# Attention score products issued half a tile ahead, with GpSimd's and the loads' order rearranged

## The reference, cut to what matters

```python
# 1. attention, 8 heads of 64: keys in a band of 96 behind the query, and the first 8 keys
scores = q @ k.T / 8 - slope[head] * dist;  scores = where(keep, scores, -1e9)
a = exp(scores - max);  x = (a / sum(a)) @ v
# 2. gated product with a causal convolution of 5 taps
gate = sigmoid(sum_k conv_w[k] * x shifted by 4 - k);  x2 = (gate * (x @ w_val)) @ w_out
# 3. x2 @ w_in (1024 wide), relu, 3 taps, gate, @ moe2_w_out (1024 x 512)
h = relu(x2 @ w_in);  out = (h * sigmoid(conv3(h))) @ w2
```

## Time and profile before

| what | value |
|---|---|
| median of 3 runs | 260.68 us (260.28 to 261.41) |
| profiled execution, its own time | 260.86 us |
| its span, first to last instruction | 259.1 us |
| busy: PE, DVE, ACT, POOL | 96%, 71%, 57%, 18% of the span |
| TensorE clock granted | full in every slice |

### The profile page before, as it was taken

One profiled execution on the slowest core, in us unless ns is written; L12 is line 12 of the kernel. 1 busy time (PEld: TensorE's weight loads), 2 busy tenths in 40 slices (PEclk: granted clock), 3 DMA queues, 4 the chain that ended last, 5 costly groups with the idle time before them and its releaser, 6 DMA issues.

```text
span 259.1 us, 4771 instructions
## 1 busy us (share of the span) xinstructions
PE 248.1 (96%) x1702; PEld 199.7 (77%) x1702; DVE 183.4 (71%) x469; ACT 147.8 (57%) x346; POOL 46.8 (18%) x71
## 2 busy tenths in 40 slices
PE   8999989989789899999999999999999999999995
PEld 7644558888688778888888888888888888888883
DVE  0388369998989988989805969986139989990000
ACT  1061649999999854455517058855458559662100
POOL 1002255777478612000000000000000000000000
PEclk9999999999999999999999999999999999999999
DMA  6799957897976120000000000000000004004021
GB/s 204 266 341 270 287 199 202 248 239 229 271 220 202 57 74 4 0 4 0 0 0 3 0 0 0 1 3 0 0 0 3 0 0 162 3 0 162 0 115 47
DMA packets 24636, 24.69 MB, mean 95 GB/s; under 512 B 3732, under 2 KB 16532, under 8 KB 24484
## 3 DMA queue, kind: packets, MB, share of 16 engines
q1 hardware_dynamic: 23460, 23.37, 29.8%
q10 hardware_dynamic: 1152, 1.01, 1.2%
HBM read 21.03 MB, written 3.34 MB: 94 GB/s over the span
## 4 chain that ended last, share of the span: by engine, by line
PE 84%; ACT 9%; DVE 5%; issue 2%
PE ps L592 21%; PE ps L594 21%; PE ps L593 21%; PE ps L478 9%; ACT prob L732 6%; PE ps L559 3%; DVE prob L982 3%; PE ps L525 2%; PE ps L563 2%; ACT probT L739 2%; PE ps L493 2%; PE ps L489 1%; DVE probT L989 1%; DVE xT L1005 1%; ACT Wh L720 0%
## 5 line engine op out<-in xcount | busy, mean ns | idle before, releaser
L732 ACT ACTIVATE prob<-prob,low 128x232 f32<-128x232 f32 (+1 forms) x96 | 44.2, 465 | 4.9 <-DVE low L982 4.8
L1010 DVE SCALAR_TENSOR_TENSOR g<-xT,cw,g 128x512 f32<-128x512 f32 x48 | 34.7, 787 | 1.6 <-ACT g L767 1.6
L838 ACT ACTIVATE h<-ps 128x512 f32<-128x512 f32 x24 | 14.0, 596 | 31.2 <-PE ps L594 31.1
L982 DVE CUSTOM_DVE_ANT_0 prob<-ps,bias 128x232 f32<-128x232 f32 x80 | 28.0, 388 | 1.5 <-PE ps L525 1.5
L559 PE MATMUL ps<-probT,v_new 128*64 128x128 f32 x192 | 19.3, 280 | 6.5 <-ACT probT L739 6.5
L592 PE MATMUL ps<-gh,Wh 128*128 128x512 f32 x64 | 24.9, 389 | 0.0
L593 PE MATMUL ps<-gl,Wh 128*128 128x512 f32 x64 | 24.9, 389 | 0.0
L594 PE MATMUL ps<-gh,Wl 128*128 128x512 f32 x64 | 24.9, 389 | 0.0
L592 PE MATMUL ps<-hghA,w2h 128*128 128x512 f32 x64 | 24.9, 389 | 0.0
L593 PE MATMUL ps<-hglA,w2h 128*128 128x512 f32 x64 | 24.9, 389 | 0.0
L594 PE MATMUL ps<-hghA,w2l 128*128 128x512 f32 x64 | 24.9, 389 | 0.0
(11 more groups left out here) (110 smaller groups left out, 590.1 us busy)
## 6 DMA issues: line engine op xcount, KB each, us to landing
q_rows<-in_q SPq DMA_DIRECT2D x12, 256.0 KB, 4.3
kW<-in_k SPq DMA_DIRECT2D x12, 256.0 KB, 5.4
v_new<-in_v SPq DMA_DIRECT2D x12, 240.0 KB
invT<-inv_turned SPq DMA_DIRECT2D x20, 128.0 KB, 3.4
out<-xT SPq DMA_DIRECT2D x5, 512.0 KB, 2.8
w<-in_w SPq DMA_DIRECT2D x8, 256.0 KB, 9.3
v_old<-in_v SPq DMA_DIRECT2D x10, 192.0 KB
prob<-in_wval SPq DMA_DIRECT2D x1, 1024.0 KB, 4.9
```

Source lines behind the costliest of these rows:

```text
L732: act.activation(part, part, ACT.Exp, scale=-1.0, bias=low[:, t % 2, i:i + 1], accum_out=total[:, t % 2, i, 0:1]).then_inc(exp_done, 1)
L838: act.activation(h_cols(m, c), pieces(HB(m), c), ACT.Relu).then_inc(relu_done, 1)
L982: dve.tensor_tensor_reduce(prob[:, t % 2, i, cols], SC(f, e)[:, i % HH // 2, cols], table, -SCALE, 3.0e38, ALU.add, ALU.min, low[:, t % 2, ...
L1010: dve.scalar_tensor_tensor(out=pieces(g[:, m, :], c), in0=x_cols(m, c, tap - PAD1), scalar=cw1[:, m, tap:tap + 1], in1=pieces(g[:, m, :], ...
```

## The change

PE computes each half of a tile's scores half a tile ahead: in iteration t, after `turn(t)`, comes the first half of `qk(t+2)`, then `pv(t)`, then the second half of `qk(t+2)`. DVE's order follows: it scores the first half of tile 1 ahead of the loop, and begins iteration t with tile t's first copy, then `inverse(t)`, the other copy, `turn_inverse(t)`, the second half of tile t+1's scores, the first half of tile t+2's, and `take_x(t)` in the same iteration. The first two taps move from ACT to GpSimd (`first_taps`, as `tensor_scalar` from SBUF to SBUF, once, in iteration 5), and DVE's early steps from iterations 8, 9, 10 to 6, 7, 10. GpSimd runs `scale_x(t-1)` ahead of `key_window(t+3)`, and splits two rows of `w2` in iterations 0 and 1, one in each of 2 to 5. SP loads rows 0 to 3 of `w2` ahead of the loop, and rows 4 to 7 behind `spread_inverse(0)` to `spread_inverse(3)`.

```diff
-EARLY_STEPS = {t: 1 for t in range(TAPS_FROM + 3, TILES - 1)}
+EARLY_STEPS = {t: 1 for t in (TAPS_FROM + 1, TAPS_FROM + 2, TILES - 2)}
+W2_FIRST = 4
+W2_ROWS = {0: (0, 1), 1: (2, 3), 2: (4,), 3: (5,), 4: (6,), 5: (7,)}
...
-                for k in range(FT):
+                for k in range(W2_FIRST):
                     load_w2(k)
...
                     spread_inverse(t)
+                    if t + W2_FIRST < FT:
+                        load_w2(t + W2_FIRST)
...
+            def first_taps():
+                pool.wait_ge(cw_in, 32)
+                pool.wait_ge(x_edges, 1)
+                pool.wait_ge(x_ready, N // P)
+                for m in range(2):
+                    pool.tensor_scalar(g[:, m, :], x_cols(m, 0, -PAD1), cw1[:, m, 0:1], None, ALU.mult).then_inc(tap0_1, 1)
...
                 for t in range(TILES):
+                    if t >= 1:
+                        scale_x(t - 1)
                     if t + 3 < TILES:
                         key_window(t + 3)
-                    if t < FT // 2:
-                        split_w2(2 * t)
-                        split_w2(2 * t + 1)
+                    for k in W2_ROWS.get(t, ()):
+                        split_w2(k)
+                    if t == TAPS_FROM:
+                        first_taps()
                     if X_SPLIT_FROM <= t < X_SPLIT_FROM + CT:
                         split_x(t - X_SPLIT_FROM)
-                    if t >= 1:
-                        scale_x(t - 1)
...
                 for t in range(TILES - 1):
-                    if t >= 1:
-                        qk(t + 1)
                     for f in range(HALVES):
                         turn(t, f)
+                    if t + 2 < TILES:
+                        qk_half(t + 2, 0)
                     pv(t)
+                    if t + 2 < TILES:
+                        qk_half(t + 2, 1)
...
-                    if t == TAPS_FROM:
-                        act.wait_ge(cw_in, 32)
-                        act.wait_ge(x_edges, 1)
-                        act.wait_ge(x_ready, N // P)
-                    if TAPS_FROM <= t < TAPS_FROM + 2:
-                        first_tap_of(0, t - TAPS_FROM)
                 copy_t0(TILES - 1, 0)
                 copy_t0(TILES - 1, 2)
+                act.wait_ge(cw_in, 32)
+                act.wait_ge(tap0_1, 2)
...
+                for i in range(HH):
+                    score(1, i)
                 for t in range(TILES - 1):
-                    if t >= 1:
-                        take_x(t - 1)
-                    score(t + 1, 0)
-                    score(t + 1, 1)
+                    copy_t1(t, 1)
                     inverse(t)
-                    score(t + 1, 2)
+                    copy_t1(t, 3)
                     turn_inverse(t)
-                    copy_t1(t, 1)
-                    score(t + 1, 3)
-                    copy_t1(t, 3)
                     for i in range(HH, H):
                         score(t + 1, i)
+                    if t + 2 < TILES:
+                        for i in range(HH):
+                            score(t + 2, i)
+                    take_x(t)
                     for _ in range(EARLY_STEPS.get(t, 0)):
                         early_conv1(next_step)
                         next_step += 1
-                take_x(TILES - 2)
```

More of the change, by code:

```diff
@@ L511, in _, with qk_half @@
             product_W(CT + 1)
+            def qk_half(t, f):
+                slot = t % RING
+                if f == 0:
+                    pe.wait_ge(q_in[slot], landed(t))
+                    pe.wait_ge(k_in[slot], landed(t))
+                    pe.wait_ge(k_window, k_windows(t))
+                if t >= 1:
+                    pe.wait_ge(score_done, H * (t - 1) + HH * (f + 1))
+                for i in range(HH):
+                    pair, rows = 2 * f + i // 2, slice(i % 2 * D, i % 2 * D + D)
+                    keys = kW[rows, slot, pair, OLD if first_of_batch(t) else 0:KEYS]
+                    last = pe.matmul(SC(f, i % 2)[:, i // 2, OLD if first_of_batch(t) else 0:KEYS], q_rows[rows, slot, pair, :], keys,
+                                     start=True, stop=True)
+                last.then_inc(qk_done, 1)
             def qk(t):
[L515 to L518, removed]
                 for f in range(HALVES):
-                    if t >= 1:
[L521 to L527, removed]
+                    qk_half(t, f)
             def turn_bank(t, j):
```

## The result

The changed kernel takes 268.49 us (median of four runs, 268.00 to 269.61) against 260.48 us of the kernel before on the same chip: a ratio of 1.0295, 95% interval 1.0271 to 1.0320. It is 8.0 us slower, outside the predicted range and beyond both of its slow rivals. The profiled execution took 268.0 us with a span of 266.2.

The account below looks back on a forecast made before the run. DVE bounds the attention stage; the look-ahead removes its 2.4 us, but the window's loop (14.75 us for three tiles) eats it: first product at 88.93, with contention 89.2 against 89.14, +0.1. Median 260.8 us, range 258.3 to 262.6.

Parts of the forecast that it names:

- the look-ahead is eaten by its own window: Attention stage: loop through SP and GpSimd takes 4.92 us a tile, replacing DVE's 4.72; range 259.4 to 262.0, chance 0.47.
- PE's idle released by the window copy and GpSimd waiting for `invT`: Signs of being right: PE idles for GpSimd's window copy in middle tiles; GpSimd waits for the inverse instead of keys.
- DVE's waits for scores: Sign of being right: DVE's waits for scores at iteration starts, 1.5 us from 36 to 89 us before, are gone.
- the slack: Key window of tile 6: done at 55.67, its product at 59.05, so 3.4 us; three edits take 4.4 us.
- Landing of the inverse at send + 7.05: Inverse's DRAM round trip: SP occupied 3.09 to 3.59 us, middle 3.35, then a read of 3.70.
- The late rows of w2: Loads in iterations 0 to 3: issue of about 0.43 us each in the sum; latency of nothing to 0.9 us a row.
- D(t+3) at window + 4.15: DVE starts iteration t+3 4.15 us behind the window: half `qk` 0.83, `pv` 1.85, half `qk` 0.83, half turn 0.55, semaphores 0.1.
- D(4): Moment DVE starts iteration 4, forecast at 56.05 us; D(t) is the same for iteration t.
- 1.24 for two taps: GpSimd, iteration 5, ahead of scaling and window: 0.62 us a tap, priced from a cast of 0.61; up to 1.28 each.
- The look-ahead's own gain: Attention stage: removes DVE's 2.4 us of waits, 0.30 a tile, leaving 4.72 us a tile instead of 5.03.
- Rival 2: Slower by DMA: w2's rows and faster pace delay keys and inverses, window at send + 10.3; +1.9, 262.6 us; chance 0.14.
- rival 3: Slower by GpSimd: taps at 1.28 us each and one DVE step at full contention; 262.8 us; chance 0.10.

Follow-up runs that it names:

- the filled kernel: The changed kernel plus nine PE products of zeros ahead of the first half of the scores of tiles 5 and 8: 268.48 us, ratio 1.0270.
- keys first: The changed kernel with GpSimd's key window of tile t+3 put back ahead of the scaling of tile t-1: 267.16 us, ratio 1.0237.
- three undone: The changed kernel with windows ahead of scalings, all of w2 loaded ahead of the loop and taps back on ScalarE: 261.62 us, ratio 1.0012.
- the deferred read: Look-ahead without the three edits; SP issues q and k first, spreads inverses one iteration later; scalings and taps later, steps in 8 to 10: 259.94 us, ratio 0.9956.

## Why the prediction was wrong

**The place was right in the changed kernel, the size was not.** The forecast was that the look-ahead is eaten by its own window, through the loop of send, spread, scaling and window. PE's idle released by the window copy and GpSimd waiting for `invT` are what it named as signs, and both are there; DVE's waits for scores, which were to vanish, grew. Two terms of the sum were too small, one lacked the clock, and the account of the slack rested on one tile: this made +0.1 of what was +7.1. And the loss doesn't need the look-ahead. Without the look-ahead's 2.2 us the forecast's account has 2.2 us taken from 3.4 and everything in time; the other edits lost 2.5% all the same.

1. **"Landing of the inverse at send + 7.05" failed.** SP's timeline of the kernel after, iteration 1:

```profile
43.05 0.56 SPq L329 DMA_DIRECT2D inv_turned<-inv_rows  x1
...
44.54 1.09 SPq L323 DMA_DIRECT2D v_old<-in_v  x1
...
46.91 1.26 SPq L337 DMA_DIRECT2D invT<-inv_turned  x2
48.21 0.60 SPq L340 DMA_DIRECT2D w<-in_w  x1
```

and what followed in the chain that ended at the late `qk`:

```profile
47.55 4.39 DMA invT<-inv_turned
...
52.17 1.12 issue
53.29 0.51 POOL kW L412
...
54.20 1.70 PE ps L537 x8
```

The send was at 43.05 (predicted 42.9). The read was issued 3.86 us later (3.35 in the sum, 3.59 the bound), since the issues themselves filled the time, one of v's with 1.09 us, and the scaling began 0.11 us behind its landing at 51.97: 5.06 us for the read against 3.70. Landing at send + 8.92. From there to the window's end 1.97 us, as the sum had it, so the window of tile 5 was done at 53.94, not at 51.9. The 3.70 came from a row at 85 us, behind the attention stage's loads; here the DMA share was 0.90 from 47 to 52 us. Both terms came from good rows of the kernel before. Its SP timeline also has 4.81 us from a write's issue to the read's:

```profile
66.59 0.56 SPq L327 DMA_DIRECT2D inv_turned<-inv_rows  x1
...
71.40 1.26 SPq L335 DMA_DIRECT2D invT<-inv_turned  x2
```

and its reads of the inverse landed 2.8 to 5.3 us behind their issue (median 3.4). The late rows of w2, bounded with 0.9 us a row and left out of the sum, are at most a part: in the kernel with the look-ahead and the scaling first, all of w2 in front, the send was at 43.14 and the scaling began at 50.99, 7.85 us later, against 9.03 here, one execution each. In the changed kernel all of w2 in front brought nothing that could be measured.

2. **"D(t+3) at window + 4.15" failed for lack of a clock term.** D(4) came 6.18 us behind the window. The half `qk` took 1.70 for 1.05, most of `pv` about one and a half times its time, and these are the windows at 0.50. In the filled kernel, at full clock, D(4) came 4.56 us behind the window (58.03 for 53.47), near the sum's 4.15: the clock's part is 1.6 us. Two such stalls (tiles 5 and 8) would make an estimated 3.2 of the 7.1 us; the filling measured one, the second is carried over from it. That is no saving to be had: with the clock kept up the whole took as long. That the clock might fall behind an idle of PE was in no rival, though the forecast itself predicted such idles.

3. **"1.24 for two taps" failed.** GpSimd's timeline from the second stall to the third:

```profile
71.43 0.21 POOL L413 COPY kW<-kW 128x32 f32<-128x32 f32 x1
71.59 0.61 POOL L425 CAST w2h<-w 128x512 fp32r<-128x512 f32 x1
72.28 1.26 POOL L427 TENSOR_TENSOR w2l<-w,w2h 128x512 fp32r<-128x512 f32 x1
73.53 3.11 POOL L442 TENSOR_SCALAR g<-xT,cw 128x512 f32<-128x512 f32 x2
76.95 1.27 POOL L419 TENSOR_TENSOR xT<-xT,invT 128x512 f32<-128x512 f32 x1 [0.32 <-DMA invT<-inv_turned]
...
78.61 0.21 POOL L413 COPY kW<-kW 128x32 f32<-128x32 f32 x1
```

Two taps took 3.11 us, beyond the upper bound of 2.56. From window 8 to window 9 it is 7.18 us, where the sum had 5.15, and the 2.0 between them is the taps' 1.87 with a wait of 0.3 for `invT`. PE's third stall follows at 79.07, with no loss of clock. What the taps cost hangs on what else is late: nothing on the kernel before, 1.1% beside the look-ahead alone, and nothing that could be measured in the changed kernel, where taking them away gave 268.81 us.

4. **"So 3.4 us was the slack" failed.** It was read at tile 6; at tile 7 the kernel before has 2.1 us (61.35 to 63.43), less than the 2.2 that the look-ahead takes by itself, and there the look-ahead alone stalled. The other users of the slack, late w2 rows and longer landings, stood in the range and the rivals one at a time. They don't come one at a time: the three edits cost 0 to 0.25% each and 2.5% together, without any look-ahead. Which two of them do it is open.

**Where the time went.** Against the forecast D(4) was 4.1 us late (60.12 for 56.05), D(6) 3.3 (69.26 for 65.95), D(7) 6.1 (76.92 for 70.8), D(8) 7.1 (83.59 for 76.5), the product 7.1. By this the two stalls and the taps hold all of it in this execution; contention of DVE's steps added nothing that shows, though one took 1.13 instead of 0.74 us.

**What held.** The look-ahead's own gain: x is taken every 4.76 to 4.84 us against 5.03 in the first tiles, whose windows were in time, in each version looked at (the kernel after, the look-ahead alone, keys first, three undone, the deferred read). That behind the stage everything is one for one: product and span both moved 7.1 us. Rival 2, slower by DMA, and rival 3, slower by the taps, each named something that is in the trace; rival 2's point of decision, a window later than send + 9.9, was passed (send + 10.9). Undone alone, neither the late w2 rows nor the taps gave back anything measurable, so neither is the cause by itself. What stays open: how the 7.1 us divide between lateness and clock over both stalls, when the clock falls and when not, why the two orders of SP's loads lost as much as they did, and what the last version owes its gain to.

## What to carry to other kernels

A look-ahead spends slack in everything that it asks for earlier, so write down the slack of each such thing and every edit that draws on the same one, and sum them before pricing any; edits that cost next to nothing singly cost 2.5% together here. Read the slack at every tile and keep the smallest. A step that waits for a round trip through DRAM does harm ahead of one that the busiest loop needs as soon as the slack is used otherwise: the scaling ahead of the window cost 0.1%, within the noise, without the look-ahead and 2.1% with it. And price an idle of PE in a stage that had none with the clock that it may cost: in the stall that was filled, 2.4 us of idle cost 1.6 us more behind it.

## What the runs showed of the hardware

- The granted clock fell to 0.50 right behind idles of PE of 2.42 and 2.43 us, and stayed full behind one of 1.71 us. In other kernels it fell about a microsecond after work had begun again, behind idles of 1.59, 1.85 and 3.35 us, and stayed full behind one of 2.26. The length of an idle alone thus doesn't tell. Nine products of zeros in the first idle of 2.4 us kept the clock full there.
- GpSimd's multiply of 128x512 by a scalar for each partition took 1.56 us, where its cast of as many elements took 0.61 and its product of two tensors 1.27. The Trainium skill, GPSIMD Engine Reference, in its side-by-side cycle accounting, gives a body of at most two operations, other than the one with two inputs, 1.03 cycles an element, and its Specifications the clock, 1.2 GHz. By that a tap would be an estimated 0.44 us without an instruction's fixed cost; the row has three and a half times as much, and the row decides.
- The same read of an inverse landed in 3.70 us behind the stage and in 5.06 and 5.25 inside it, in two of the kernels; the write of one took 4.38 us in one of them.
